# A recurrence's input loads laid in DRAM in parts with gaps, so that a row is two or four packets

## What is computed

```python
# stage 1: r, k, v, w, a, b have shape (B, H, S, D) = (4, 8, 768, 40), float32
for t in range(S):
    y[:, :, t] = einsum('bhd,bhde->bhe', rt, state)
    Sa = einsum('bhde,bhe->bhd', state, at)
    state = state * wt[:, :, None, :] - einsum('bhd,bhe->bhde', Sa, bt) \
          + einsum('bhd,bhe->bhde', vt, kt)
# stage 2: x = y laid out as (B, S, H*D) -> relu(x @ w_in), 3-tap conv, sigmoid gate, @ w_out
# stage 3: per expert: q, k, v projections, causal softmax, top-2 weights, @ wo, summed
```

## Time and profile before

| what | value |
|---|---|
| median of 3 runs | 922.32 us (921.68 to 924.01) |
| the profiled execution's own time | 932.08 us |
| its span, first to last instruction | 930.3 us |
| TensorE (PE) busy | 825.4 us, 89% of the span |
| DVE, ACT, POOL busy | 557.9, 317.4, 264.5 us |
| DMA moved | 61.33 MB in 130,506 packets |
| TensorE's granted clock over the span | 0.945 of full speed |

### The profile page before, as it was taken

How to read it: one execution, slowest core, us unless ns; L and a number is a source line. 1 busy time by engine, 2 the same in 40 slices (tenths; PEclk the granted TensorE clock), 3 DMA queues, 4 the chain that set the end, 5 groups by cost and what they waited for, 6 DMA issues and landing times.

```text
span 930.3 us, 27678 instructions
## 1 busy us (share of the span) xinstructions
PE 825.4 (89%) x11872; PEld 597.4 (64%) x11872; DVE 557.9 (60%) x1222; ACT 317.4 (34%) x741; POOL 264.5 (28%) x537
## 2 busy tenths in 40 slices
PE   2536899988999988889998899999999988999988
PEld 2436889888998988874455654555645555555555
DVE  8893968968698732126537735347455367363474
ACT  4101323323232322123226632236532256322364
POOL 2078787878778767000000000000000000000000
PEclk9999988978697988699999999988999999999999
DMA  3544756666567563622100000100000000000000
GB/s 107 140 105 88 145 133 143 142 155 137 126 146 134 119 154 86 144 56 62 43 1 8 22 15 1 43 0 16 22 8 25 18 8 16 22 1 0 1 15 30
DMA packets 130506, 61.33 MB, mean 66 GB/s; under 512 B 106128, under 2 KB 119376, under 8 KB 130384
## 3 DMA queue, kind: packets, MB, share of 16 engines
q1 hardware_dynamic: 95740, 32.61, 16.1%
q10 hardware_dynamic: 34644, 26.95, 10.9%
HBM read 45.37 MB, written 14.16 MB: 64 GB/s over the span
## 4 chain that ended last, share of the span: by engine, by line
PE 70%; POOL 7%; DVE 7%; DMA 5%; ACT 5%; issue 5%; SPq 1%; ACTq 0%; DVEq 0%
PE ps_all L769 8%; PE ps_all L753 8%; PE ps_all L879 5%; PE ps_all L813 5%; PE ps_all L861 4%; PE ps_all L891 4%; PE ps_scan L189 4%; POOL solver_then_w_down L328 4%; POOL t_update L326 3%; PE ps_scan L106 3%; PE ps_scan L131 3%; PE ps_all L756 3%; PE ps_all L763 2%; PE ps_all L796 2%; PE ps_scan L168 2%
## 5 line engine op out<-in xcount | busy, mean ns | idle before, releaser
L326 POOL TENSOR_TENSOR t_update<-solver_then_w_down 128x110 f32<-128x110 f32 (+17 forms) x257 | 121.1, 471 | 87.7 <-DVE solver_then_w_down L328 68.0
L328 POOL TENSOR_TENSOR solver_then_w_down<-solver_then_w_down,t_update 128x110 f32<-128x110 f32 (+17 forms) x257 | 134.3, 523 | 20.1
L106 PE MATMUL ps_scan<-decayed_a_and_eye,scaled_then_x 40*128 40x104 f32 x768 | 67.6, 345 | 36.8 <-DVE decayed_a_and_eye L360 36.8
L1090 DVE TENSOR_REDUCE minus_max<-ps_all 128x1 f32<-128x128 f32 (+5 forms) x96 | 55.3, 618 | 66.7 <-PE ps_all L865 66.7
L769 PE MATMUL ps_all<-gated,solver_then_w_down 128*128 128x384 f32 x256 | 91.1, 499 | 0.0
L753 PE MATMUL ps_all<-scaled_then_x,inputs_then_w_up 128*128 128x384 f32 x256 | 88.8, 490 | 1.8 <-ACT ak_l_then_ffn L931 1.8
L106 PEld LDWEIGHTS ps_scan<-decayed_a_and_eye,scaled_then_x 40*128 40x128 f32 x768 | 62.8, 252 | 38.9 <-issue 37.9
L989 ACT ACTIVATE probs_t<-ps_all 128x512 f32<-128x512 f32 (+3 forms) x128 | 55.1, 452 | 70.0 <-PE ps_all L879 69.3
L769 PEld LDWEIGHTS ps_all<-gated,solver_then_w_down 128*128 128x128 f32 x256 | 46.0, 189 | 44.6 <-issue 19.1
L753 PEld LDWEIGHTS ps_all<-scaled_then_x,inputs_then_w_up 128*128 128x128 f32 x256 | 47.5, 190 | 36.4 <-ACT ak_l_then_ffn L931 6.0
L233 ACT ACTIVATE x_rhs<-ps_scan 128x320 f32<-128x320 f32 x48 | 21.0, 438 | 143.3 <-PE ps_scan L123 71.3
(11 more groups left out here) (116 smaller groups left out, 1519.9 us busy)
## 6 DMA issues: line engine op xcount, KB each, us to landing
r_t_and_v_t<-in_rv ACTq DMA_DIRECT2D x48, 160.0 KB
inputs_then_w_up<-in_x ACTq DMA_DIRECT2D x46, 160.0 KB
solver_then_w_down<-l_blocks SPq DMA_DIRECT2D x24, 256.0 KB, 4.6
uv_and_ruv<-in_v ACTq DMA_DIRECT2D x48, 80.0 KB, 3.4
y_t<-y_out SPq DMA_DIRECT2D x24, 160.0 KB
out<-out_rows SPq DMA_DIRECT2D x24, 160.0 KB, 1.8
inputs_then_w_up<-in_x ACTq DMA_DIRECT2D x46, 81.4 KB
inputs_then_w_up<-in_x ACTq DMA_DIRECT2D x46, 80.0 KB
```

The costliest lines, as they stand in the source:

```text
L106: last = nc.tensor.matmul(PS[:, o:o + ROWS], weights, AL[c % NK][rows(h), p, :], start=True, stop=True)
L326: return (lambda: eng.tensor_tensor(tmp[:, 0:cols, 0:rest], l[:, s:s + 1, s + 1:BLK].broadcast_to(shape), t[:, 0:cols, s:s + 1].broadcast_ ...
L328: lambda: eng.tensor_tensor(t[:, 0:cols, s + 1:BLK], t[:, 0:cols, s + 1:BLK], tmp[:, 0:cols, 0:rest], ALU.subtract))
L1090: nc.vector.tensor_reduce(NM[:, v:v + 1], PS[:, first_bank(v) * 512:first_bank(v) * 512 + n], AX.X, ALU.min).then_inc(m["nm"], 1)
```

## The change

The DRAM array in_x becomes three arrays, in_w, in_a and in_kb, and each row of them, and of in_rv, is cut into 2, 2, 4 and 4 parts, with 8 unused floats (32 bytes) behind each part. A load of 40 rows then has 80 pieces of 1040 ("w") or 1024 bytes ("a"), or 160 pieces of 1024 bytes ("kb" and in_rv), where before it had 40. The tiles in SBUF are what they were. Column 520 isn't loaded any more: it is set to zero by a memset, and so each of the two memsets of INX becomes three; on POOL each of the three is waited for.

```diff
+PARTS_OF = {"w": 2, "a": 2, "kb": 4}
+GAP = 8
-PARTS = {"w": slice(0, WCOLS + 1), "a": slice(WCOLS + 1, WCOLS + 1 + HC), "kb": slice(WCOLS + 1 + HC, XCOLS)}
+PARTS = {"w": slice(0, WCOLS), "a": slice(WCOLS + 1, WCOLS + 1 + HC), "kb": slice(WCOLS + 1 + HC, XCOLS)}
...
+    def pieces(n, h, part):
+        return INX[n][rows(h), PARTS[part]].rearrange("r (s c) -> r s c", s=PARTS_OF[part])
+
+    def from_dram(c, h, part):
+        src = {"w": in_w, "a": in_a, "kb": in_kb}[part]
+        return src[c, h][:, :, 0:src.shape[-1] - GAP]
...
-                act.dma_start(INX[c % 2][rows(h), PARTS[part]], in_x[c, h][:, PARTS[part]]).then_inc(m[f"{part}{c % 2}"], 16)
+                act.dma_start(pieces(c % 2, h, part), from_dram(c, h, part)).then_inc(m[f"{part}{c % 2}"], 16)
...
-                act.dma_start(RV[n % 3][rows(h), :, :, :].rearrange("r k p t -> r (k p t)"),
-                              in_rv[n, h].rearrange("r k p t -> r (k p t)")).then_inc(m[f"r{n % 3}"], 16)
+                act.dma_start(RV[n % 3][rows(h), :, :, :].rearrange("r k (s q) t -> r (k s) (q t)", s=2),
+                              in_rv[n, h][:, :, 0:HC // 2]).then_inc(m[f"r{n % 3}"], 16)
-        act.wait_ge(m["set_inx1"], 1)
+        act.wait_ge(m["set_inx1"], 3)
...
-        nc.vector.memset(INX[0][BLK:C, :], 1.0).then_inc(m["set_inx"], 1)
+        nc.vector.memset(INX[0][:, WCOLS:WCOLS + 1], 0.0)
+        nc.vector.memset(INX[0][BLK:C, WCOLS + 1:XCOLS], 1.0)
+        nc.vector.memset(INX[0][BLK:C, PARTS["w"]], 1.0).then_inc(m["set_inx"], 1)
...
-        nc.gpsimd.memset(INX[1][BLK:C, :], 1.0).then_inc(m["set_inx1"], 1)
+        nc.gpsimd.memset(INX[1][:, WCOLS:WCOLS + 1], 0.0).then_inc(m["set_inx1"], 1)
         pool.wait_ge(m["set_inx1"], 1)
+        nc.gpsimd.memset(INX[1][BLK:C, PARTS["w"]], 1.0).then_inc(m["set_inx1"], 1)
+        pool.wait_ge(m["set_inx1"], 2)
+        nc.gpsimd.memset(INX[1][BLK:C, WCOLS + 1:XCOLS], 1.0).then_inc(m["set_inx1"], 1)
+        pool.wait_ge(m["set_inx1"], 3)
...
-                sp.dma_start(INX[0][rows(h), PARTS[part]], in_x[0, h][:, PARTS[part]]).then_inc(m[f"{part}0"], 16)
+                sp.dma_start(pieces(0, h, part), from_dram(0, h, part)).then_inc(m[f"{part}0"], 16)
...
+    def apart(x, parts):
+        x = x.reshape(NT, 2, D, parts, -1)
+        return np.concatenate([x, np.zeros(x.shape[:-1] + (GAP,), np.float32)], -1)
+
-    return {"in_x": x, "in_v": np.ascontiguousarray(vn),
-            "in_rv": np.ascontiguousarray(np.stack([split(r), split(v)], 3))}
+    return {"in_w": apart(ws, PARTS_OF["w"]), "in_a": apart(split(a), PARTS_OF["a"]), "in_kb": apart(kb, PARTS_OF["kb"]),
+            "in_v": np.ascontiguousarray(vn), "in_rv": apart(np.stack([split(r), split(v)], 3), 4)}
```

More of the change, by code:

```diff
@@ L30, with recurrence @@
 BEGUN = 16
-PARTS = {"w": slice(0, WCOLS + 1), "a": slice(WCOLS + 1, WCOLS + 1 + HC), "kb": slice(WCOLS + 1 + HC, XCOLS)}
-def recurrence(nc, sem, in_x, in_v, in_rv, l_dram, t_dram, y_t, inputs, scaled, solver, products,
+PARTS = {"w": slice(0, WCOLS), "a": slice(WCOLS + 1, WCOLS + 1 + HC), "kb": slice(WCOLS + 1 + HC, XCOLS)}
+def recurrence(nc, sem, in_w, in_a, in_kb, in_v, in_rv, l_dram, t_dram, y_t, inputs, scaled, solver, products,
                load_weights, load_w_down, load_early_tokens, load_late_tokens, first_product):
@@ L1162, in feed_forward_and_attention, with build @@
     return ctx, program, up
-def build(nc, in_x, in_v, in_rv, w_in, conv_w, w_out, w_qk, w_vg, w_o, out):
+def build(nc, in_w, in_a, in_kb, in_v, in_rv, w_in, conv_w, w_out, w_qk, w_vg, w_o, out):
     with ExitStack() as top:
@@ L1204, in first_product @@
             up(pe, 0, (xt_late, 16 * (KF + 1)))
-        ctx, first, meet = recurrence(nc, sem, in_x, in_v, in_rv, l_dram, t_dram, y_t, inputs, scaled, solver, products,
+        ctx, first, meet = recurrence(nc, sem, in_w, in_a, in_kb, in_v, in_rv, l_dram, t_dram, y_t, inputs, scaled, solver, products,
                                       load_weights, load_w_down, load_early_tokens, load_late_tokens, first_product)
```

## The result

The kernel after took 932.0 us, median of 7 runs (928.11 to 935.17), against 923.93 us for before (7 runs, 917.31 to 928.43): ratio 1.008, interval 1.0047 to 1.0113. It is slower by 6 to 8 us, where I had forecast +1.45, and outside my range.

The account below looks back on a forecast made before the run. Bound: DVE, DMA and POOL to 77 us, TensorE (PE) from 190, changing hands between. 0.34 + 0.58 + 0.29 - 0.4 + 0.64 = +1.45 us on 922.32 gave 923.8 us; range 921 to 925.5, 8 in 10 916.5 to 927.5.

Parts of the forecast that it names:

- step 7: Issuing each load: +38 ns, upper bound +284; hidden at the start, later covered by 2.98 us of slack on ACT: nothing.
- Ten engines: Loads of 40 rows stay on ten DMA engines after the change, giving 49,604 packets on ACT's queue; forecast's chance 0.57.
- step 1: DVE's memset becoming three: +0.12 us, hidden because the ten engines are by then busy with ACT's loads.
- step 2: POOL's memset becoming three with two more waits: ACT's first loads start later, +0.34 us on the chain.
- step 4: l_out at 26.53 us, beside the loads of chunk 4: about 36 more packets, +0.29 us.
- Step 3: The start: 72 more packets on each engine before chunk 0's "kb" lands, +0.58 us; bk waits for it.
- Step 5: l_in at 32.50 us, beside chunk 5's loads: +0.29 for packets, -1.2 if queues take turns by packet; taken as -0.4 us.
- rival B: Faster: SP's packets wait for shorter ones on ten shared engines, -3.0 us, 919.3 us; chance 0.07 by more than 0.3%.
- Step 6: t_out and t_in at 123 and 180 us: 40 more packets, 0.32 us each time, +0.64 us; nothing at 70.
- Step 8: The rest of the 15,360 added packets, behind 190 us: hidden by PE's matmuls, no cost.
- A: Rival, faster: loads spread over 16 engines, shortening the start, l_in and late trips, -5.5 us, 916.8 us; chance 0.12.
- C: Rival, slower: added packets dearer, 25.0 ns each, at the start and on SP's trips, +5.9 us, 928.3 us; chance 0.24.

Follow-up runs that it names:

- run 1: Kernel after with one more 32-byte gap ahead of each DRAM row, so both sides are 40 rows of 2 or 4 parts: 924.64 us, ratio 0.9997 to before.
- run 6: Kernel before with two small DMAs behind each load of "w" and "a" alone, from step 0 on: 959.27 us, ratio 1.0345 to before.
- run 7: Kernel before with small DMAs behind the loads of "kb" and in_rv alone: 924.75 us, ratio 1.0007 to before.
- run 11: Kernel of run 6 with three matmuls on the identity ahead of TensorE's wait for x_rhs in each step: ratio 1.0051 to before, median 938.24 us.
- run 5: Kernel after, unchanged, measured again beside before on the same chip: 931.89 us, ratio 1.0061 to before.
- run 4: Kernel before with only the change's memsets, three on DVE and three on POOL with their waits: 923.62 us, ratio 0.9977 to before.
- run 12: Kernel before with two matmuls on the identity ahead of TensorE's wait for x_rhs in each step: 930.12 us, ratio 1.0033 to before.
- run 3: Kernel before with loads of in_x and in_rv made 48 rows, on 16 engines: 936.16 us, ratio 1.0117 to before.
- runs 1 to 10: The first ten follow-up kernels, variants of before or after without added filling matmuls: ratios to before from 0.9977 to 1.0345.

## Why the prediction was wrong

**The step that failed is step 7, the issue time**, and in it two things. The price: I took +38 ns, from a store whose two sides have the same 40 rows of 8 pieces, with 284 ns as the upper bound from in_v, and measured +421 on in_x's median issue. The store's sides are alike; in_v's are not (its DRAM side has no gaps, its SBUF side is 64 rows of 8 pieces), and yet it is no bound for this pair. The change makes the sides of 40-row loads unlike, and run 1, which makes them alike again, has the old issue time and no loss. I had seen that no row had such a pair and used this for the number of engines, where it didn't matter, and not for the issue, where it did.

The place: I called the stretch from ZS to bk_natural the tightest one on ACT, with 2.98 us of slack. That was one step at half clock. Runs 6 and 7 show the tight place to be the one ahead of x_rhs, whose slack at full clock is 1.3 us (a hole of 2.75, 1.44 of it in use). Four issues of 773 ns are 3.1 us.

**The price of a short wait** is in none of my steps. I took a wait on TensorE as costing its length. Here its length was the smaller part; what followed was half clock for some 10 us. I had said that another clock than 0.83 from 190 us on would make me wrong altogether. It was 0.85 there, but from 77 to 190 it was 0.88 where before's profile had 0.94. That idle TensorE brings the clock down, and that this is most of run 6's price, is shown by run 11. For the kernel after itself the means of run 5's set point the same way: its executions ran longer at half clock, by about two standard errors, and span times clock is before's. Its two profiles alone would not show it: both have 0.86 over the recurrence, no lower than the long one of before. In run 5's profile such a pause stands some 2 us ahead of a fall:

```profile
105.33 1.13 PE L142 MATMUL ps_scan<-x_rhs,block_inverse_t 64*64 64x40 f32 x32 [0.77 <-ACT x_rhs L244]
```
```profile
90.40:107.30 16.90, 16.00 (x548) 15.19 (x540) 14.96 (x27) 4.73 (x11) 11.38 (x20) 1.00 0.65 141
107.40:114.10 6.70, 6.70 (x98) 6.13 (x96) 3.52 (x6) 1.83 (x4) 5.89 (x11) 0.50 1.03 172
```

No run puts the filling matmuls into the kernel after, so that its own pauses bring the clock down is argued, not shown.

**Ten engines** was right: 49,604 packets. **Steps 1, 2 and 4** were right or harmless. POOL's memsets cost 0.31 us until ACT's first issue (2.63 to 2.94), against 0.34:

```profile
0.80 0.10 POOL L464 MEMSET inputs_then_w_up<- 104x1 f32 x1 [0.29 <-POOLq L1292]
0.95 0.53 POOL L466 MEMSET inputs_then_w_up<- 32x520 f32 x1
1.54 1.38 POOL L468 MEMSET inputs_then_w_up<- 32x1536 f32 x1
```

**Step 3**, the start: bk began at 13.19 us (13.03 in run 5's profile), I had said 12.6. It began at 12.68 in run 1, with cheap issues, and at 12.69 in run 4, with the memsets alone, and at 11.7 to 12.3 in kernels that start as before does, so step 7's share is at most some 0.5 us, no more than that scatter. ACT's six first issues took 5.5 us and pushed its table load and the copies of the eyes back, which I had called hidden; the chain of after runs through them until 21 us.

**Step 5**, l_in, went the way of rival B and further than I took. L_in's first pair landed 7.5 us after its second issue in before and 5.3 us in after, -2.2 against my -0.4. (The Trainium skill, "DMA: Bandwidth & Descriptors", queues, rings and completion order, has an engine change queues at packet ends, but its packet is a group of several descriptors, and no run separates such turn-taking from the loads' later issue.) Part of the 2.2 us is scatter: the same piece took 6.49 to 6.88 us in runs 6, 11 and 12, which load as before does there. It paid back the start: the first matmul behind x_rhs ran at 77.2 against 77.5 us. **Step 6** had +0.32 for each late trip; the t_out pieces went from 5.5 to 3.9 and from 5.6 to 6.6 us, so no steady sign. **Step 8**, packets hidden behind 190: right, by run 1.

**The rivals.** A fell twice: the loads stayed on ten engines, and run 3 shows no gain from 16. C had the right sign and a chance of 0.24, and the wrong mechanism: run 1 has all of C's packets and no cost. My sign was right, by luck, and the size four to six times too small: the terms that made up my +1.45, memsets and packets, cost nothing that runs 4 and 1 can show.

## What to carry to other kernels

A DMA's layout has a price on the queue that issues it, apart from what the DMA engines do. Keep both sides' dimensions alike, here by one gap that breaks the even pitch of DRAM's pieces, and read the issue time of each DMA form before and after. Then ask, in a step at full clock, which waits lie behind these issues: a queue can take 52 us more where it has holes, and 1.7 us more a step at the wrong one cost 6 to 8 us. And where TensorE's clock already falls to half now and then, a short wait can cost several times its length: in run 6 some 7 us of waits went with a loss of 33.

## What the runs showed of the hardware that was not expected

- Of DMAs with 40 rows, ACT issued one in 287 (the shortest) to 384 ns (the longest median) with 40 rows of 1, 2 or 4 pieces on both sides, and in 773 to 801 ns with DRAM as 80 or 160 pieces at one pitch and SBUF as 40 rows of 2 or 4. Before's trace has what may be a milder case on SP, which I had read and left out: t_out, 1024 pieces against 64 rows, 620 ns, where l_in's plain 64 rows take 556. Unlike sides alone therefore don't give the size of it.
- 15,360 more packets, of 1024 bytes in place of a quarter or half as many cost nothing within 0.4%.
- In the first loads sixteen DMA engines moved 181 GB/s with 48 rows and ten moved 178 with 50 (155 with 40): engine time for a byte was half as long again on sixteen. Busy engines don't prove that engines are the limit.
- Over the twelve profiles with the same matmuls (before, after, runs 1 to 10) the recurrence took 327 to 366 us, and length times clock 288 to 298. Pauses of 0.8 and 0.9 us at 2.4 GHz stood ahead of 7 and 10 us at 1.2.
